# Both rewrites at once: a reordered end of attention, ELU stage and weight loads, and an output stage with one 512-column matmul per k tile

## What is computed

```python
kv = einsum('bhsd,bhse->bhde', k, v); out = einsum('bhsd,bhde->bhse', q, kv)   # 8 x 8 heads, 576 x 64
x = out / sqrt(mean(out * out, -1) + 1e-6) * g_norm                            # then (4608, 512)
x = (sigmoid(x @ w_gate) * (x @ w_val)) @ w_out        # 512 -> 1536 -> 512
h = x @ w_in                                           # 512 -> 2048
out = where(h > 0, h, exp(min(h, 0)) - 1) @ w_out2     # ELU, 2048 -> 512
```

## Time and profile before

| | |
|---|---|
| time, median of 3 runs | 1703.28 us (1703.05 to 1709.16) |
| the profiled execution | 1700.83 us, span 1698.7 us |
| TensorE | 1639.0 us busy, 96% of the span |
| VectorE | 1198.8 us, 71% |
| ScalarE | 819.1 us, 48% |
| GpSimd | 181.7 us, 11% |
| moved by DMA | 339.35 MB, mean 200 GB/s |

### The profile page before, as it was taken

The page is one execution under the profiler, slowest core; times in us unless marked ns, Lnnn a source line. Parts: engine busy times, 40 slices in busy tenths (PEclk is TensorE's granted clock), DMA queues, the critical chain, the costliest instruction groups (busy, mean ns, idle before and its releaser), DMA issues.

```text
span 1698.7 us, 27990 instructions
## 1 busy us (share of the span) xinstructions
PE 1639.0 (96%) x10920; PEld 1613.1 (95%) x10920; DVE 1198.8 (71%) x1429; ACT 819.1 (48%) x1251; POOL 181.7 (11%) x185
## 2 busy tenths in 40 slices
PE   6996999999999999999999999999999899999999
PEld 5776999999999999999999999999999799999999
DVE  5777888887588754777777666776765676766764
ACT  6664555554455443444444444554454444444443
POOL 6564222220022100000000000000000000000000
PEclk9998999999999999999999999999999999999999
DMA  9993488878788456554333754423329833333341
GB/s 279 283 293 130 161 309 314 311 292 318 257 302 313 175 180 228 206 226 142 137 137 140 284 193 140 149 105 138 139 103 347 300 128 125 125 124 125 133 145 55
DMA packets 194745, 339.35 MB, mean 200 GB/s; under 512 B 13376, under 2 KB 149568, under 8 KB 194624
## 3 DMA queue, kind: packets, MB, share of 16 engines
q1 hardware_dynamic: 194624, 337.69, 56.6%
HBM read 191.89 MB, written 145.75 MB: 199 GB/s over the span
## 4 chain that ended last, share of the span: by engine, by line
PE 75%; DVE 6%; ACT 4%; issue 4%; DMA 2%; SPq 1%; POOL 0%; ACTq 0%; DVEq 0%; POOLq 0%
PE pair L898 38%; PE pair L963 21%; PE pair L931 15%; DVE s L1393 3%; DVE e L1498 2%; ACT e L1187 1%; DMA u_elu<-s 1%; ACT s L1206 1%; ACT e L1223 1%; ACT e L1218 1%; DMA wreg<-weight_items 1%; DMA weight_items<-out_w 0%; ACT s L1197 0%; ACT ring L1083 0%; SPq L493 0%
## 5 line engine op out<-in xcount | busy, mean ns | idle before, releaser
L898 PE MATMUL pair<-ring,wreg 128*128 128x384 f32 x5040 | 887.7, 337 | 25.5 <-ACT s L1206 15.5
L898 PEld LDWEIGHTS pair<-ring,wreg 128*128 128x128 f32 x5040 | 879.7, 189 | 32.6 <-ACT s L1206 20.9
L963 PE MATMUL pair<-wreg,ring 128*128 128x256 f32 x3024 | 364.8, 284 | 6.6 <-DMA wreg<-weight_items 6.6
L963 PEld LDWEIGHTS pair<-wreg,ring 128*128 128x128 f32 x3024 | 364.6, 193 | 6.8 <-DMA wreg<-weight_items 6.8
L1393 DVE TENSOR_TENSOR s<-s,pair 128x768 f32<-128x768 f32 (+1 forms) x252 | 210.7, 836 | 179.4 <-PE pair L898 144.3
L931 PE MATMUL pair<-ring,wreg 128*128 128x384 f32 x1512 | 262.2, 334 | 0.0
L931 PEld LDWEIGHTS pair<-ring,wreg 128*128 128x128 f32 x1512 | 262.1, 188 | 0.0
L1317 DVE TENSOR_TENSOR ring<-raw,ring 128x1024 fp32r<-128x1024 f32 (+1 forms) x162 | 180.7, 1134 | 112.3 <-ACT ring L1093 97.3
L1187 ACT ACTIVATE e<-e 128x768 f32<-128x768 f32 x72 | 61.0, 847 | 185.9 <-DVE e L1498 185.9
L1093 ACT ACTIVATE ring<-raw 128x1024 fp32r<-128x1024 f32 x108 | 111.8, 1051 | 55.7 <-DVE raw L1351 41.3
L1317 DVE TENSOR_TENSOR ring<-sum,ring 128x768 fp32r<-128x768 f32 (+1 forms) x90 | 92.3, 1038 | 30.2 <-ACT ring L1093 13.5
(11 more groups left out here) (98 smaller groups left out, 1475.5 us busy)
## 6 DMA issues: line engine op xcount, KB each, us to landing
wreg<-weight_items SPq DMA_DIRECT2D x98, 512.0 KB, 6.8
raw<-u_elu SPq DMA_DIRECT2D x36, 1024.0 KB, 7.4
u_gated<-ub SPq DMA_DIRECT2D x144, 192.0 KB, 2.8
u_elu<-s SPq DMA_DIRECT2D x72, 384.0 KB, 2.4
weight_items<-out_w SPq DMA_DIRECT2D x50, 512.0 KB, 4.6
weight_items<-out_x SPq DMA_DIRECT2D x48, 512.0 KB, 4.7
x_raw<-x_attention SPq DMA_DIRECT2D x48, 384.0 KB, 5.2
raw_k<-u_gated SPq DMA_DIRECT2D x6, 2304.0 KB, 8.4
```

The lines of the kernel that those rows point to most:

```text
L898: mm = pe.matmul(dst[:, g, 0:NT], w[:, a, cols], ring[:, slot, b, kt, :], start=(i in STARTS and kt == a == b == 0), stop=(kt == 1 and a = ...
L963: mm = pe.matmul(dst[:, 0, 0:256], s[:, b, 2 * c + kt, :], w[:, a, cols], start=(i in STARTS and c == kt == a == b == 0), stop=(c == 3 and ...
```

## The change

- Output stage: for each k tile the high activations are multiplied by the high and low weights in one matmul of 512 columns into a whole PSUM bank; the low activations by the high weights go, 256 columns, onto the bank's second half. Snapshots and combines become 512 columns wide, and VectorE adds the two halves at the end (`fold`) before the store.
- ELU stage: a second set of result buffers (s1b, s5b, s2b) for even units, so a snapshot waits for the store of the unit before the last. The split of P1 for the next group of units moves from the last unit of a group to the one before. Output weights are loaded a unit earlier, as the products of the same unit release them; the second raw input's first half moves to the last ELU unit.
- End of attention: x is loaded four pairs earlier, its sums and two of its splits are done before the last pairs, GpSimd's sums for weight chunk 1 are spread over pairs 25 to 34, ScalarE copies P1 and P6 of unit 0 within its attention program, TensorE makes P6 right after P2, and unit 0 has an order of its own on ScalarE and VectorE. Squares and factors change places in SBUF.

The diff's core, in the order of the file; `exp`, `minimum` and `result` of the ELU stage and `combine` are as before but for the buffer they name, `gate`, `sigmoid` and `copy_p1` to `copy_p5` are the lines of `gated_unit` as functions.

```diff
@@ -186,7 +186,10 @@
         with ExitStack() as stack:
             (raw_12,) = view(stack, [("raw_12", [P, 6, NT], F32, 24 * KIB)])
         with ExitStack() as stack:
-            e_3 = view(stack, [
+            s1b, s5b, s2b, *e_3 = view(stack, [
+                ("s1b", [P, 2, NT], F32, 69 * KIB),
+                ("s5b", [P, 2, NT], F32, 72 * KIB),
...
+                ("s1_4", [P, 2, 256], F32, 87 * KIB),
+                ("s2_4", [P, 2, 256], F32, 89 * KIB),
+                ("s5_4", [P, 2, 256], F32, 91 * KIB),
+                ("c21_4", [P, 2, 256], F32, 93 * KIB),
...
+        def parts3(n):
+            return {"11": s1b, "12": s2b, "22": s5b} if n % 2 == 0 else {"11": s1, "12": s2, "22": s5}
...
+        def wide(pair_of_banks):
+            return pair_of_banks[:, 0, :].rearrange("p (a c) -> p a c", a=2)
...
+                sp.wait_ge(s_fold, folded(n, c))
...
-                if p == PAIRS - NP:
+                if p == PAIRS - RING:
                     for m in range(RING):
                         sp.wait_ge(s_xst[m], 16)
                     load_x(x1_dram, 0)
...
                     if j == 1 and at == 0 and last:
                         load_raw4(0)
-                    if j > 0 and at == 0 and last:
-                        sp.wait_ge(s_prod, prod(n - 1, P4))
-                    if j == 2 and at == 0 and last:
+                    if n == FIRST4 - 1 and at == 2:
+                        for m in range(4):
+                            sp.wait_ge(s_st[m], 16 * n)
                         load_raw4(1, (0,))
                     pieces = ((0, 1), (2, 3), (4, 5), (6,))[at]
                     if n < FIRST3 + 2:
                         load_unit_items(IN + 2 + n - FIRST3, BUF3[2 + n - FIRST3], pieces)
-                    if last and j > 0:
-                        load_out_cells(BUF3[j - 1], pieces)
+                    if last and at > 0:
+                        items = ((0, 1), (2, 3, 4), (5, 6))[at - 1]
+                        if n < FIRST4 - 1:
+                            sp.wait_ge(s_prod, prod(n, items[-1]))
+                            load_out_cells(BUF3[j], items)
+                        elif at < 3:
+                            sp.wait_ge(s_prod, prod(n, items[-1]))
+                            load_out_cells(BUF3[j], items)
                     store_elu(n, c)
             sp.wait_ge(s_prod, prod(FIRST4 - 1, P4))
-            load_out_cells(BUF3[3], range(4))
             for c in range(2):
                 sp.wait_ge(s_st[c], 16 * FIRST4)
             load_raw4(1, (1,))
-            load_out_cells(BUF3[3], range(4, 7))
+            load_out_cells(BUF3[3], (5, 6))
 
             for vis in range(NR):
...
-            static_steps(step, PAIRS - RING, PAIRS + LM + 1)
-            for c in range(1, CHUNKS):
+            static_steps(step, PAIRS - RING, PAIRS - RING + 2)
+            weight_sums(1, (0,))
+            static_steps(step, PAIRS - RING + 2, PAIRS - RING + 3)
+            weight_sums(1, (1,))
+            static_steps(step, PAIRS - RING + 3, PAIRS - RING + 4)
+            weight_sums(1, (2,))
+            static_steps(step, PAIRS - RING + 4, PAIRS + LM + 1)
+            weight_sums(1, (3,))
...
-                        for b, a in PARTS:
-                            mm = pe.matmul(dst[:, 0, 0:256], s[:, b, 2 * c + kt, :], w[:, a, cols],
-                                           start=(i in STARTS and c == kt == a == b == 0),
-                                           stop=(c == 3 and kt == 1 and b == 1),
-                                           skip_group_check=i not in STARTS)
+                        pe.matmul(dst[:, 0, :], s[:, 0, 2 * c + kt, :], w[:, :, cols],
+                                  start=(i in STARTS and c == kt == 0), stop=False, skip_group_check=True)
+                        mm = pe.matmul(dst[:, 0, 256:512], s[:, 1, 2 * c + kt, :], w[:, 0, cols],
+                                       start=False, stop=(c == 3 and kt == 1), skip_group_check=True)
...
             gated_product(0, P2)
-            static_steps(step, PAIRS + 3, PAIRS + 4)
             gated_product(0, P6)
-            static_steps(step, PAIRS + 4, PAIRS + 5)
+            static_steps(step, PAIRS + 3, PAIRS + 5)
...
+            def first_unit():
+
+                copy_p5(0)
+                fill1(0, 0)
+                fill1(0, 1)
+                sigmoid(0, "11")
+                fill1(0, 2)
+                sigmoid(0, "22")
+                fill1(0, 3)
+                fill1(0, 4)
+                sigmoid(0, "12")
+                fill1(0, 5)
+                fill1(0, 6)
+                sigmoid_c21(0)
...
-                elif j == UNITS3 - 1 and vis + 1 < NS:
+                elif j == UNITS3 - 2 and vis + 1 < NS and i == 6:
+                    split_x2(vis + 1, P1)
+                elif j == UNITS3 - 1 and vis + 1 < NS and i > 0:
...
-                act.wait_ge(s_st[2], 16 * n)
-                act.activation(s2[:, :, :], pa[:, :, 0:NT], ACT.Copy).then_inc(s_snap, 1)
+                act.wait_ge(s_st[2], 16 * (n - 1))
+                if n == FIRST3 + 1:
+                    act.wait_ge(s_st[0], 16 * FIRST3)
+                act.activation(part["12"][:, :, :], pa[:, :, 0:NT], ACT.Copy).then_inc(s_snap, 1)
                 fill3(n, 3)
                 act.wait_ge(s_prod, prod(n, P5))
-                act.wait_ge(s_st[1], 16 * n)
-                act.activation(s5[:, :, :], PB[:, :, 0:NT], ACT.Copy).then_inc(s_snap, 1)
+                act.wait_ge(s_st[1], 16 * (n - 1))
...
-                        act.activation(s5_4[:, :], PB[:, 0, 0:256], ACT.Copy).then_inc(s_snap, 1)
+                        if vis == 0:
+                            act.wait_ge(s_st[3], 16 * n)
+                        act.activation(s5_4[:, :, :], wide(PB), ACT.Copy).then_inc(s_snap, 1)
...
-                for i in {PAIRS - 1: (P1, P2), PAIRS: (P6,), PAIRS + 2: (P5,), PAIRS + 3: (P7,), PAIRS + 4: (P3,),
-                          PAIRS + 5: (P4,)}.get(p, ()):
+                if p == PAIRS + 1:
+                    act.wait_ge(s_ms, PAIRS)
+                    copy_p1(0)
+                if p == PAIRS + 3:
+                    copy_p6(0)
+                for i in {PAIRS - 4: (P1,), PAIRS - 3: (P2,), PAIRS: (P6,), PAIRS + 1: (P5,), PAIRS + 2: (P7,),
+                          PAIRS + 3: (P3,), PAIRS + 4: (P4,)}.get(p, ()):
                     split_x1(0, i)
-            act.wait_ge(s_ms, PAIRS)
-            act.wait_ge(s_rlo, B)
-            for n in range(FIRST2):
+            first_unit()
+            for n in range(1, FIRST2):
...
+            def first_unit():
+
+                combine(0, "11", s1[:, :, :], PC[:, :, 0:NT])
+                combine(0, "22", s5[:, :, :], PA[0][:, :, 0:NT])
+                fill1(0, 0)
+                fill1(0, 1)
+                gate(0, "11")
+                fill1(0, 2)
+                gate(0, "22")
+                combine(0, "12", s2[:, :, :], PB[:, :, 0:NT])
+                fill1(0, 3)
+                fill1(0, 4)
+                gate(0, "12")
+                fill1(0, 5)
+                fill1(0, 6)
+                gate_c21(0)
...
+            def fold(n, c):
+
+                if c == "21":
+                    dve.wait_ge(*c21_taken(n))
+                else:
+                    dve.wait_ge(s_comb, comb(n, c))
+                acc = {"11": s1_4, "12": s2_4, "22": s5_4, "21": c21_4}[c]
+                dve.tensor_tensor(acc[:, 0, :], acc[:, 0, :], acc[:, 1, :], ALU.add).then_inc(s_fold, 1)
+
...
+                    if i == 1 and vis > 0:
+                        fold(n - 1, "21")
+                    if i - 1 == P2:
+                        fold(n, "11")
+                    if i - 1 == P7:
+                        fold(n, "22")
+                    if i - 1 == P3:
+                        fold(n, "12")
...
-                for name in {PAIRS - 2: ("S3", "S2"), PAIRS + 1: ("S1",), PAIRS + 2: ("S4",)}.get(p, ()):
-                    sum_x(1, 0, name)
-                for i in {PAIRS - 1: (P1, P2), PAIRS: (P6,), PAIRS + 2: (P5,), PAIRS + 3: (P7,), PAIRS + 4: (P3,),
-                          PAIRS + 5: (P4,)}.get(p, ()):
+                if PAIRS - 7 <= p < PAIRS - 3:
+                    sum_x(1, 0, SUMS[p - (PAIRS - 7)])
+                for i in {PAIRS - 4: (P1,), PAIRS - 3: (P2,), PAIRS: (P6,), PAIRS + 1: (P5,), PAIRS + 2: (P7,),
+                          PAIRS + 3: (P3,), PAIRS + 4: (P4,)}.get(p, ()):
                     split_x1(0, i)
-            for n in range(FIRST2):
+            first_unit()
+            for n in range(1, FIRST2):
```

173 lines of the change are left out of this document (96 added, 77 removed).

## The result

The changed kernel took 1682.88 us (median; single runs 1679.23, 1679.24, 1686.52 and 1687.9), the kernel before 1703.16 beside it: a ratio of 0.9875, interval 0.9858 to 0.9891. By that interval it is faster, as forecast, but by 20 us and not by 45, and the median lies 8 us above the upper end of the range (1675).

A forecast was written before the change was run, and what follows sets the result against it. TensorE is busy 96% of the span, so only its idle time, low clock or shorter matmuls pay. 13.7 + 8.1 + 7.8 + 16.1 - 0.7 = 45.0 us gained gave 1658.3 us, range 1650 to 1675.

The forecast's parts named there:

- The price of a matmul: Output stage: 13.6 ns fixed per instruction, so a pair takes 346.4 ns instead of 360.0; 13.7 us gained.
- The slower rival: Output stage: second run of 256 in the 512 columns streams at half rate, pair 453 ns, kernel 1766 us; chance 0.03.
- The end of the kernel: After the last product, copy, fold and store follow one another; 0.7 us lost.
- Start of the output stage: Earlier weight loads cut the 6.6 us weight wait and the low clock after it; 8.1 us gained, ends 4 and 8.6.
- the cover: First output unit: the P5 copy's new wait for the last c21 store is hidden, the store landing near 1334, needed by 1338.
- steady part: ELU stage, groups of four units: moving the split of P1 gains 0.13 us five times, 0.7 us.
- the sum of 7.8: ELU stage: gains at the start, in the steady state and at the end together 7.8 us; ends 3 and 24.
- the start's clock term: Start of the ELU stage: 1.3 us gained from less low clock behind the first P7 stall.
- End of attention: Early copies and moved x work let unit 1 begin at 163.3 instead of 179.4: 16.1 us gained, ends 8 and 19.
- the delay of the loop: Attention's last pairs: moved work and loads delay the loop by 3 us, ends 0 and 7, so it ends at 140.4.
- the free run of unit 1: End of attention: unit 1 runs without a stall, chunk 2 of the weights landing near 161, just in time for ScalarE.
- the end of attention clogs: Rival: x loads delay q and k, sums delay kv copies, chunk 2 late; only 4 of 16 us, 1670; chance 0.09.

The follow-up runs named there:

- the kernel of 1675 us: The 1679.31 us kernel, its first output unit changed: P6's copy not waiting for quarter 12's store, P5's copy buffer moved, weight cells 0 to 3 earlier; 1675.38 us.

## Why the prediction was wrong

**The price of a matmul: right in its mechanism, with luck in the number.** In the profile of the kernel after the product ends are 2.77 us apart and the pair costs 346.7 ns, as the line through the two widths gave; the fixed part is per instruction. The slower rival, two runs of 256 as one moving operand, did not come: the 512 columns are followed after 0.23 us. Not foreseen was the second pace, 6.6 ns above it, 6.7 us a run when drawn early. Seven of eleven profiles have it, and for them the term is worth 6.7 us and not 13.4; two of the four runs of the kernel after may owe their 7 to 8 us to it, which only a profile of them could show. VectorE did not hold the stage: no wait for a combine in the kernel after.

**The end of the kernel: right**, 0.7 us.

**Start of the output stage: the step that failed is the cover.** 2.9 us came of 8.1. The stores of unit 65 were taken to land in time for every copy, and only the P5 copy's new wait was asked about; that one is hidden, as forecast. The weights did come in time too. But P6's copy waited for quarter 12's store until 1332.9. I had summed the bytes behind 1325 for the weights, and not asked what the cells moved ahead do to the stores that a copy waits for. With that wait taken away, in the kernel of 1675 us, no stop over 0.4 us is left there.

**ELU: steady part and start about right, its end wrong.** Of the 7.8 us, 1.7 came. Four units take 60.76 us (1002.07 to 1062.83) instead of 60.9, P7's first wait is 0.40 instead of 3.22. The start gave 4.1 us of 4.8, the steady part 0.5 of 0.7; the end, from the last steady stall at 1245.18 us on, lost 2.9 where 2.3 were to be gained. The step that failed is the sum of 7.8: it took the start's and the end's gains and set nothing against them. Unit 63 was given 2 MB of input beside seven weight cells; a store took 10.95 us, and a wait of 3.50 us with 3.0 us of low clock ate most of the gains. That the loads are the cause is shown: with them spread the stage takes 368.3 us, 4.9 less than before; the wait of 1.99 us left there is the one that the prediction let stay. The other 2.9 of the 7.8 don't come even so: the end gains 0.5 us instead of 2.3 there, with a new wait of 0.64 us for a P1 copy in it, and the start's clock term gave less than its 1.3. That part is open.

**End of attention: the delay of the loop and the free run of unit 1 fell.** 4.2 us came of 16.1. The prediction named its own sign: "I am wrong if ... the loop ends after 144".

First, the delay of the loop was taken at 3 us with ends 0 and 7; it ended 9.1 us later than before, at 146.5 instead of 137.4, above the end of 7. From there on the forecast path held: unit 1 began 22.2 us behind the loop's end where 22.9 had been reckoned (the prediction's 14.7 us of VectorE work add up to 14.4, which changes nothing). So it began at 168.70 instead of 163.3, still 10.5 us earlier than before. Behind that point part of the delay is paid back, since the kv wait of 1.79 us of the earlier trace rows and its low clock are gone: the first gated product starts 5.0 us later than before, and from first to last reciprocal the loop lost 4.3.

What the delay is made of is only in part known. VectorE stood 2.4 us for the x tile with all kv copies behind it, TensorE waited 4.76 and 1.93 us, and its granted clock was 0.77 from 120 to 135 us and 0.89 from 135 to 150; but with that stand taken away by later sums the loop was as long. Of the 4.3 us, leaving out the sums' width took 1.8, and putting loads, sums and splits back took 1.3 to 3.5 (four profiles); the rest is open.

Second, unit 1 was taken to run without a stall. It takes 21.4 us instead of 14.6: 3.7 us of waits and 2.9 of low clock. The splits of chunk 1 follow the x work on both engines, and GpSimd's sums of chunk 2, whose load the forecast called "just in time", slow VectorE by a factor of 2.5. This is shown: without those sums the wait of 3.1 us is gone. A busy time for each engine was in the sum, the slowing of one by the other wasn't.

Third, "what is moved still has to be done" stands in the text, and yet the move of the x work was given a gain: putting it back or spreading it changed the sum by no more than profiles of the same code differ.

The rival *the end of attention clogs* (4 of 16 us, chance 0.09) has the size that came, and its sign of late kv copies; it and the two losses at the stores came together, where the range took such things one at a time.

**Open.** Why a break of the stream leaves TensorE at one spacing or the other wasn't found; shown is only that stops draw it and that the order of the two widths changes the pattern. What sets the first 34 to 42 us wasn't tried.
